# A two-layer kernel behind chunked attention: the first chunk's keys and values early, queries decayed by VectorE, states read by ScalarE

## The reference

```python
# q, k, v: 2 x 8 heads x 768 tokens x 64, float32
gamma = 1.0 - 2.0 ** (-5.0 - np.arange(H))
for t in range(S):
    state = gamma[None, :, None, None] * state + np.einsum('bhd,bhe->bhde', k[:, :, t], v[:, :, t])
    y[:, :, t] = scale * np.einsum('bhd,bhde->bhe', q[:, :, t], state)
# x = y as 1536 tokens x 512
h = x @ w_in                                # 512 -> 2048
x = (h * (1.0 / (1.0 + np.exp(-1.702 * h)))) @ w_out
rms = np.sqrt(np.mean(x * x, axis=-1, keepdims=True) + 1e-06)
xn = x / rms * rms_g
g = xn @ w_gate                             # 512 -> 1536
out = (g * (1.0 / (1.0 + np.exp(-g))) * (xn @ w_val)) @ w_out2
```

## Time and profile before

| | us |
|---|---|
| median of 3 runs | 584.25 |
| lowest and highest | 584.05, 584.41 |
| the profiled execution | 583.44 |
| its span, first to last instruction | 581.6 |
| TensorE busy in the span | 573.3 (99%) |
| VectorE, ScalarE, GpSimd busy | 359.2, 298.1, 172.1 |

### The profile page before, as it was taken

One profiled execution on the slowest core, in us unless ns is written; L12 is line 12 of the kernel. 1 busy time (PEld: TensorE's weight loads), 2 busy tenths in 40 slices (PEclk: granted clock), 3 DMA queues, 4 the chain that ended last, 5 costly groups with the idle time before them and its releaser, 6 DMA issues.

```text
span 581.6 us, 9400 instructions
## 1 busy us (share of the span) xinstructions
PE 573.3 (99%) x3640; PEld 551.8 (95%) x3640; DVE 359.2 (62%) x486; ACT 298.1 (51%) x501; POOL 172.1 (30%) x222
## 2 busy tenths in 40 slices
PE   7999999999999999999999999999999999999997
PEld 7988999999999999999999999998889999998886
DVE  5797555676425667775346768678755666666432
ACT  1244766645336766645237655574444555564321
POOL 2386444000222452000314464410051545420000
PEclk9999999999999999999999999999999999999999
DMA  8981222322112222312202222233213322224202
GB/s 319 392 292 37 74 72 73 108 73 73 38 36 73 72 74 70 111 39 72 73 0 74 73 74 72 74 84 99 73 36 125 93 73 73 73 74 112 69 1 108
DMA packets 24220, 52.84 MB, mean 91 GB/s; under 512 B 1776, under 2 KB 1904, under 8 KB 24176
## 3 DMA queue, kind: packets, MB, share of 16 engines
q1 hardware_dynamic: 23600, 50.41, 28.2%
q10 hardware_dynamic: 576, 1.84, 0.8%
HBM read 49.09 MB, written 3.15 MB: 90 GB/s over the span
## 4 chain that ended last, share of the span: by engine, by line
PE 97%; DVE 1%; DMA 1%; issue 0%; ACT 0%
PE bank L539 20%; PE twin L539 20%; PE twin L480 11%; PE twin L483 11%; PE twin L482 11%; PE bank L483 6%; PE bank L480 6%; PE bank L482 6%; PE twin L392 2%; PE bank L438 2%; PE bank L425 1%; DMA arena<-attn_in 1%; PE bank L409 1%; DVE x_lo L787 0%; PE bank L580 0%
## 5 line engine op out<-in xcount | busy, mean ns | idle before, releaser
L778 DVE TENSOR_TENSOR w_lo<-raw,w_hi 128x512 fp32r<-128x512 f32 (+2 forms) x148 | 149.3, 1024 | 49.7 <-ACT w_hi L612 49.5
L1059 POOL TENSOR_TENSOR raw<-raw 128x256 f32<-128x256 f32 x40 | 32.1, 803 | 317.1 <-DMA raw<-w 312.5
L480 PE MATMUL twin<-x_hi,w_hi 128*128 128x384 f32 x360 | 120.5, 335 | 0.6 <-ACT arena L676 0.6
L483 PE MATMUL twin<-x_hi,w_lo 128*128 128x384 f32 x360 | 120.3, 334 | 0.0
L482 PE MATMUL twin<-x_lo,w_hi 128*128 128x384 f32 x360 | 120.2, 334 | 0.0
L612 ACT ACTIVATE w_hi<-raw 128x512 fp32r<-128x512 f32 (+2 forms) x148 | 109.0, 763 | 18.0 <-PE bank L539 7.6
L813 DVE TENSOR_TENSOR g_lo<-arena,g_hi 128x768 fp32r<-128x768 f32 x56 | 54.3, 970 | 74.8 <-ACT g_hi L642 74.8
L642 ACT ACTIVATE g_hi<-arena 128x768 fp32r<-128x768 f32 x56 | 47.5, 848 | 103.6 <-PE bank L539 103.6
L480 PEld LDWEIGHTS twin<-x_hi,w_hi 128*128 128x128 f32 x360 | 67.6, 188 | 0.9 <-ACT arena L676 0.9
L482 PEld LDWEIGHTS twin<-x_lo,w_hi 128*128 128x128 f32 x360 | 67.6, 188 | 0.0
L483 PEld LDWEIGHTS twin<-x_hi,w_lo 128*128 128x128 f32 x360 | 67.6, 188 | 0.0
(11 more groups left out here) (105 smaller groups left out, 995.9 us busy)
## 6 DMA issues: line engine op xcount, KB each, us to landing
raw<-w SPq DMA_DIRECT2D x68, 512.0 KB, 3.7
arena<-attn_in SPq DMA_DIRECT2D x22, 512.0 KB, 7.9
out<-x SPq DMA_DIRECT2D x1, 1536.0 KB, 8.6
out<-x SPq DMA_DIRECT2D x6, 256.0 KB, 2.0
arena<-attn_in ACTq DMA_DIRECT2D x2, 512.0 KB, 10.1
arena<-tables ACTq DMA_DIRECT2D x1, 512.0 KB, 6.1
arena<-tables ACTq DMA_DIRECT2D x1, 256.0 KB, 9.8
ident<-ident_in SPq DMA_DIRECT2D x1, 64.0 KB, 12.8
```

What stands on the lines that cost most here:

```text
L480: pe.matmul(dst, w_hi[q][:, w], x_hi[:, x], start=start and kk == 0, stop=False, skip_group_check=True)
L483: mm = pe.matmul(dst, w_lo[q][:, w], x_hi[:, x], start=False, stop=kk == 1, skip_group_check=True)
L778: dve.tensor_tensor(w_lo[q % 3][:, dst], src, w_hi[q % 3][:, dst].bitcast(F32), ALU.subtract)\
L1059: pool.tensor_tensor(s1, a21, a22, ALU.add).then_inc(w_sums, 1)
```

## The change

The first chunk's queries come on SP's queue and its keys on ScalarE's, each 256 KB, and its keys and values in token order second on SP's; `load_kv(1)` and `load_kv(2)` change queues. Chunk 0 is finished (from_chunk, new_products) ahead of scores(1), with 12 fill matmuls before it in place of 3. `decay_q` is VectorE's for all chunks, right behind `masked`. `new_state` is ScalarE's: one instruction for chunks 0 and 6, and for the others four, one for each pair of heads. It stands ahead of `copy_y` and of most conversions in ScalarE's order. In the first hidden unit product 6 stands ahead of product 3, the split of T4 behind copy_u2, and the sum for T4 in the last attention round. Left out below are hunks that only rename a semaphore or write a wait's value by a helper.

```diff
--- before.py
+++ after.py
@@ -23,7 +23,7 @@
 NF1, NF2 = FF1 // P, FF2 // P
 EPS = 1e-6
 WARM_UP = 8
-FILL = 3
+FILL = 12
 T_MASK = HEADS + PAIRS
@@ -52,7 +52,7 @@
 UPPER = {True: (B11, B21, B22, T1, T3, T2, T4), False: (B11, B21, T1, T2, B22, T3, T4)}
-LOWER = {True: (B11, B21, T1, B22, T3, T2, T4), False: (B11, B21, T1, T2, B22, T3, T4)}
+LOWER = {True: (B11, B21, T1, B22, T2, T3, T4), False: (B11, B21, T1, T2, B22, T3, T4)}
 SET = ((0, 1, 2), (3, 4, 5))
...
@@ -318,6 +318,13 @@
                 ins = engine.memset(state_decay[64 * (h % 2):64 * (h % 2) + 64, at_:at_ + 1], gamma(h) ** (CHUNK * c))
             return ins
+        def qk_at(a):
+
+            return 16 * (a // SLOTS) + (32 if a % SLOTS == 0 else 16)
+
+        def kv_at(a):
+            return 16 * (a // SLOTS) + 16
+
         block = ctx.enter_context(nc.Block())
         @block.sync
@@ -339,9 +346,10 @@
                 sp.dma_start(dst, src).then_inc(raw_in[r % 2], 16)
-            load(0)
+            sp.dma_start(slot[0][:, 0:512], attn_in[0, :, 0:512]).then_inc(qk_in[0], 16)
+            load_kv(0)
             load(1)
-            load_kv(1)
+            load_kv(2)
             load(2)
             load(3)
             load_kv(3)
@@ -353,11 +361,13 @@
                     sp.wait_ge(scores_done, b - SLOTS + 1)
                     if (b - SLOTS) % CHUNKS > 0:
-                        g, c = chunk_of(b - SLOTS)
-                        sp.wait_ge(q_decayed[g], c)
+                        sp.wait_ge(q_decayed, cross_at(b - SLOTS) + 1)
                     load(b)
                 for b in (a, a + 1):
                     sp.wait_ge(y_done, b - SLOTS + 1)
+                    if b == SLOTS:
+
+                        sp.wait_ge(kv_done, 1)
                     load_kv(b)
                 if a == 8:
                     load_weights(1)
...
@@ -430,8 +439,7 @@
             def from_chunk(a):
                 par = a % 2
                 v = slot[a % SLOTS][:, 1536:2048]
-                if a % CHUNKS == CHUNKS - 1:
-                    pe.wait_ge(kv_in[a % SLOTS], 16 * (a // SLOTS) + 16)
+                pe.wait_ge(kv_in[a % SLOTS], kv_at(a))
                 pe.wait_ge(probs_done, a + 1)
                 for p in range(PAIRS):
                     for h in range(2):
@@ -442,19 +450,21 @@
                 mm.then_inc(y_done, 1)
             pe.wait_ge(ones_set, 1)
-            for _ in range(WARM_UP):
-                pe.matmul(gate[1][:, 0:P], ones[:, :], ones[:, :], start=True, stop=True)
+            def fill(count):
+
+                for _ in range(count):
+                    pe.matmul(gate[1][:, 0:P], ones[:, :], ones[:, :], start=True, stop=True)
+
+            fill(WARM_UP)
             for a in range(0, STEPS, 2):
                 scores(a)
                 if a == 0:
-
-                    for _ in range(FILL):
-                        pe.matmul(gate[1][:, 0:P], ones[:, :], ones[:, :], start=True, stop=True)
+                    fill(FILL)
+                    from_state(0)
+                    from_chunk(0)
+                    new_products(0)
                 scores(a + 1)
                 if a == 0:
-                    new_products(0)
-                    from_state(0)
-                    from_chunk(0)
                     from_state(1)
                     new_products(1)
                 else:
@@ -514,9 +524,9 @@
                     pe.wait_ge(m1_copied, n + 1)
                     product(2, n, 0, 0, 2, B21, False)
                     pe.wait_ge(w_lo_done, lo_at[r] + 2)
+                    product(6, n, 2, 1, 2, T2, False)
                     pe.wait_ge(m5_copied, n + 1)
                     product(3, n, 1, 1, 3, B22, False)
-                    product(6, n, 2, 1, 2, T2, False)
                 pe.wait_ge(u2_copied, n + 1)
                 pe.wait_ge(w_lo_done, lo_at[r] + 3)
                 product(7, n, 2, 1, 0, T3, False)
@@ -685,10 +695,10 @@
                    .then_inc(squared, 1)
+            act.dma_start(slot[0][:, 512:1024], attn_in[0, :, 512:1024]).then_inc(qk_in[0], 16)
             act.dma_start(mask, tables[:, T_MASK:T_Q]).then_inc(mask_in, 16)
-            act.dma_start(slot[0][:, 1024:2048], attn_in[0, :, 1024:2048]).then_inc(kv_in[0], 16)
             act.dma_start(q_table, tables[:, T_Q:T_ALL]).then_inc(q_table_in, 16)
-            act.dma_start(slot[2][:, 1024:2048], attn_in[2 * BATCH, :, 1024:2048]).then_inc(kv_in[2], 16)
+            act.dma_start(slot[1][:, 1024:2048], attn_in[BATCH, :, 1024:2048]).then_inc(kv_in[1], 16)
             act.wait_ge(ones_set, 1)
             act.activation(warm[:, :], ones[:, 0:1], ACT.Gelu_apprx_sigmoid)
@@ -700,6 +710,24 @@
                                gate[a % 2][:, :].rearrange("p (d k t) -> p d k t", d=2, k=2),
                                ACT.Copy).then_inc(y_copied, 1)
+            def new_state(a):
+                g, c = chunk_of(a)
+                if c == CHUNKS - 1:
+                    return
+                m = state_at(a)
+                act.wait_ge(kv_done, m + 1)
+                if m >= 2:
+                    act.wait_ge(cross_done, m - 1)
+                if c == 0:
+                    ins = act.activation(state[m % 2], val[g][:, 0:256], ACT.Copy)
+                else:
+                    for p in range(PAIRS):
+                        at_ = PAIRS * c + p
+                        ins = act.activation(state[m % 2][:, cols(p, 64)], val[g][:, cols(p, 64)], ACT.Copy,
+                                             scale=state_decay[:, at_:at_ + 1])
+                ins.then_inc(state_done, 1)
+
+            act.wait_ge(factors_set, 2)
             for a in range(0, STEPS, 2):
                 if a == 4:
                     split_x(0, B11)
@@ -709,13 +737,21 @@
                     split_x(0, B22)
                     split_w(0, 1)
                 elif a == 8:
-                    split_x(0, T1)
                     split_x(0, T3)
                     split_w(0, 2)
-                elif a == 10:
+                if a == 0:
+                    copy_y(0)
+                    new_state(0)
+                new_state(a + 1)
+                if a > 0:
+                    copy_y(a)
+                copy_y(a + 1)
+                if a + 2 < STEPS:
+                    new_state(a + 2)
+                if a == 6:
+                    split_x(0, T1)
+                elif a == 8:
                     split_x(0, T2)
-                copy_y(a)
-                copy_y(a + 1)
             for p, (layer, _) in enumerate(PHASES):
@@ -730,10 +766,10 @@
                     copy_m5(n)
                     if j > 0 and not is_val(n - 1):
                         activate(n - 1, 3)
+                    split_next(r, 0)
+                    copy_u2(n)
                     if n == 0:
                         split_x(0, T4)
-                    split_next(r, 0)
-                    copy_u2(n)
                     if not is_val(n):
                         activate(n, 0)
                     split_next(r, 1)
@@ -896,61 +932,39 @@
                 dve.tensor_tensor(prob[a % 2], twin[a % 2][:, :], mask, ALU.mult)\
                    .then_inc(probs_done, 1)
-            def new_state(a):
-                g, c = chunk_of(a)
-                if c == CHUNKS - 1:
-                    return
-                m = state_at(a)
-                dve.wait_ge(kv_done, m + 1)
-                if m >= 2:
-                    dve.wait_ge(cross_done, m - 1)
-                if c == 0:
-                    ins = dve.tensor_copy(state[m % 2], val[g][:, 0:256])
-                else:
-                    new, sums = (t.rearrange("p (k e) -> p k e", k=PAIRS) for t in (state[m % 2], val[g][:, 0:256]))
-                    ins = dve.tensor_tensor(new, sums, state_decay[:, cols(c, PAIRS)].unsqueeze(2).to_broadcast([P, PAIRS, 64]), ALU.mult)
-                ins.then_inc(state_done, 1)
-
             def decay_q(a):
-
                 r, x = a % SLOTS, cross_at(a)
                 if a == 1:
                     dve.wait_ge(q_table_in, 16)
-                dve.wait_ge(qk_in[r], 16 * (a // SLOTS) + 16)
+                dve.wait_ge(qk_in[r], qk_at(a))
                 if x >= 2:
                     dve.wait_ge(cross_done, x - 1)
-                dve.tensor_tensor(q_dec[x % 2], slot[r][:, 0:512], q_table, ALU.mult).then_inc(q_decayed[0], 1)
+                dve.tensor_tensor(q_dec[x % 2], slot[r][:, 0:512], q_table, ALU.mult).then_inc(q_decayed, 1)
             for a in range(0, STEPS, 2):
                 masked(a)
                 if a == 0:
                     decay_q(1)
-                    new_state(0)
                 masked(a + 1)
-                if a < 4:
-                    decay_q(a + 2)
-                elif a == 4:
+                for b in (a + 2, a + 3):
+                    if b < STEPS and b % CHUNKS > 0:
+                        decay_q(b)
+                if a == 4:
                     lower_x(0, B11)
-                elif a == 8:
-                    lower_x(0, T1)
```

(37 more changed lines are left out.)

## The result

| | before | after |
|---|---|---|
| median us (15 executions each) | 584.31 | 586.88 |
| lowest and highest | 583.52, 585.33 | 585.02, 590.36 |
| profiled execution, its span | 583.44, 581.6 | 585.10, 583.3 |
| TensorE, VectorE, ScalarE, GpSimd busy | 573.3, 359.2, 298.1, 172.1 | 574.3, 356.1, 306.0, 164.9 |

Ratio 1.0048, 95% interval [1.0037, 1.0059]: slower by 2.6 us, where 1.1 was forecast, and 0.1 us above the stated range. The profiled execution lies at the fast end and shows 1.7 of it. The 15 executions are not one cloud: those with a mean granted TensorE clock of 1.000 took 585.0 to 586.4, those with 0.997 took 586.5 to 588.4, those with 0.994 took 589.0 to 590.4. The medians of the three groups are 585.5, 587.2 and 589.6.

What follows compares the result with a forecast made beforehand. The prediction took TensorE's nearly gapless matmul stream as the bound, with key arrivals pinning the attention stage. Stage -0.2 and first unit +1.3 gave +1.1 us, 584.5 profiled, 0.8 more for the median: 585.3 us, range 583.0 to 586.8.

Steps and rivals of the forecast that it cites:

- The start: First chunk: scores from 5.2 us, clock rise at about 11.1, fills end at 11.7, chunk 2's scores at 17.1.
- The first chunk early: 0: Attention start: finishing the first chunk early changes the time by 0, ends -0.3 and +0.8 us.
- a gain is waited away: At chunk 4's keys: their arrival doesn't move, so TensorE's earlier time becomes waiting; a delay up to 0.34 us is absorbed.
- Rival 1: Attention stage: transfers come sooner, chunk 10's keys over 1.3 us before 42.54, stage -1.4 to -2.7, middle 583.5; chance 0.21.
- Rival 2: Attention start: too many fills, ending at 12.4, stage 0.8 us late, total +2.1, 586.3; chance 0.15.
- States and queries: Attention stage: states on ScalarE save the 0.28 us wait at 32.87 and 0.1 restart; queries on VectorE gain 0.1.
- The term that decides: First hidden unit: unit 1 waits for its weights and starts at 59.1 against 57.79, 1.3 us lost; ends 0.7 and 1.8.
- the T4 pair: First hidden unit, VectorE: lowering T4, then the next unit's first weights, taken as 2.48 us together.
- Rival 3: First hidden unit: the new wait isn't there, the unit saves 0.84 us, total 583.2; chance 0.09.
- The sum: Whole kernel: stage -0.2 and first unit +1.3 give +1.1 us, profiled execution 584.5, median 585.3.
- the median of the runs stands 0.8 above it: Last step: the median lies 0.8 us above the profiled execution, so 584.5 becomes 585.3.

Runs made afterwards that it cites:

- e1: The changed kernel with ScalarE's split of T4 put back before unit 1's first weight split and copy_u2: 583.98 us, ratio 1.0005.
- e4: The changed kernel with 3 fill matmuls instead of 12: 585.44 us.
- e8: The kernel before with product 6 ahead of product 3 in the first unit and nothing else: 583.42 us, ratio 0.9988.
- e6: The changed kernel with VectorE lowering unit 1's first weights ahead of T4: 583.75 us, ratio 0.9991.
- e3: The kernel before with product 6 ahead of product 3 and the split of T4 behind copy_u2: 585.57 us.
- e9: The changed kernel with one more 768-column VectorE subtraction ahead of the lowering of T4, lengthening the wait before unit 1: 589.18 us.
- e7: The changed kernel with the split of T4 put back and five idle matmuls each ahead of the products of chunks 4 and 10: 584.02 us.
- e10: The changed kernel with idle matmuls in all three long waits, nine ahead of unit 1, five each at chunks 4 and 10: 586.13 us.
- e11: The changed kernel with unit 1's weights lowered ahead of T4 and five idle matmuls each at chunks 4 and 10: 584.08 us, ratio 1.0002.
- e2: The changed kernel with nine idle matmuls before the wait for unit 1's w_lo: 585.67 us.
- e5: The changed kernel as it is, measured again as a yardstick on another chip: 585.89 us.

## Why the prediction was wrong

*The start.* The place of the scores was right (5.18 for 5.2), the clock wasn't. I let it rise at 11.1. The 24 fill records took 2.94 us, the same as in e1's profile, where the scores ahead of them already ran at the upper level (16 records in 1.16 us); so all of them ran at that level, the rise came by about 7.2, and the fills ended at 10.1 instead of 11.7. What stands between them and the scores of chunk 2 took 6.3 us (10.06 to 16.34) where I had 5.4, with waits of 0.20 and 0.24 us in it. The two errors partly cancel, which is luck. The step itself ("The first chunk early: 0") held because "a gain is waited away": the keys of chunk 4 absorbed it. Rival 1 fell, since chunk 10's keys came 0.34 us later and not sooner. Rival 2 fell with the fill end at 10.1, and e4 with three fills starts the scores of chunk 2 no sooner.

*States and queries.* Four state reads took 0.93 us for my 1.0, and the wait at 32.87 went. But one of the same size took its place. VectorE, with its conversions now ahead, comes 0.85 us later to the masks of chunks 6 and 7, and the from-chunk matmuls wait for it; before (first line) and after:

```profile
32.65 2.34 DVE L896 TENSOR_TENSOR arena<-twin,arena 128x1024 f32<-128x1024 f32 x2
```

```profile
33.50 2.34 DVE L932 TENSOR_TENSOR arena<-twin,arena 128x1024 f32<-128x1024 f32 x2
...
34.86 2.23 PE L446 MATMUL bank<-arena 128*64 128x128 f32 x32 [0.35 <-DVE arena L932]
```

By chunk 10's products TensorE was 0.74 us later than before (ready at 43.79 for 43.05), and the wait for the keys swallowed nearly all of it. The keys came at 42.88, 0.34 later than before, were decayed in 1.12 us for 1.38, and the stage ended 0.17 later, not 0.2 earlier.

In other profiles that decay is slower. In the new order it starts together with a pair of VectorE conversions; its rows, from e8 (order of before) and from e1 (order of the change):

```profile
43.09 1.04 POOL L1044 TENSOR_TENSOR arena<-arena 128x512 f32<-128x512 f32 x1 [2.77 <-DMA arena<-attn_in]
```

```profile
43.37 1.83 POOL L1057 TENSOR_TENSOR arena<-arena 128x512 f32<-128x512 f32 x1 [5.70 <-DMA arena<-attn_in]
```

Over the profiles it took 1.04, 1.04, 1.25 and 1.38 us in the old order and 1.05 to 1.83 in the new one. It also starts later: at 42.95 on average over four profiles of the old order, 43.39 over ten of the new. With the boundary clean on both sides and no idle matmuls, one pair compares the attention stages: 583.75 (e6) against 583.42 (e8), with intervals that overlap. So the changed stage is worth nothing; whether it costs a few tenths of a microsecond, and by which of the two, isn't shown.

*The first unit.* The term that decides was right in kind and in size: 1.3 forecast, 1.35 measured. Inside it two small errors cancelled, the T4 pair at 2.73 us for 2.48 and a restart of 0.06 us behind it for my 0.24. e1, e3 and e6 confirm the chain from three sides. Rival 3 fell.

*The sum.* For the profiled execution 584.5 was forecast and 585.10 came: 0.6 short, 0.4 of it from the stage and 0.14 from behind the boundary, where nothing was forecast. The failed step is the next one, "the median of the runs stands 0.8 above it": after the change it stood 1.8 above (586.88 against 585.10). The 0.8 was the distance of a kernel without a long pause in its matmuls; by carrying it over I priced the wait at its length alone and put the clock behind it at nothing, without a reason. What stood in its place is a second price, **some 1.6 us for each fall of TensorE's clock behind an idle wait**. By times and clocks it was paid in nine of fifteen executions, and about twice in three of them. I had looked at the clock only as something that rises once at the start; no rival let it fall. The Trainium skill ("TensorE: Matmul & The Clock Gate", What's actually happening) names falls after idleness, and I used none of it. In e4 a pause of 1.77 us went before one.

How far that is shown: e4 and e9 show the fall in its place and its cost in time; e7, e10 and e11 show none where the waits are filled or gone. That a longer wait brings more falls is only suggested by e9. e2, with only the boundary filled, still had one execution of eight at 588.1, and e1 three of twelve with only the key waits left, so the 1.2 to 1.7 us waits at chunks 4 and 10 probably take part; which of the waits caused which fall of the first measurement stays open, since only profiled executions show the place, and its own has no fall. In e5, with three executions of ten under clock 0.998, the same kernel took 585.89, 1.6 us above before and inside the range: there the forecast would have held by luck, with the same price missing.

## What to carry to other kernels

Before moving an instruction behind a copy, follow everything queued behind it on the next engine too: here a ScalarE edit delayed VectorE's first instruction in line and with it a second, unrelated one that TensorE waited for. Where TensorE never pauses, price a new pause of about 2 us twice, its length and the chance of a spell at half clock behind it. Where it can't be avoided, fill it with idle matmuls, but with fewer than the wait holds: at chunk 10 they overran the keys by about 1 us in e10's and e11's profiles. And a gain ahead of a wait for a transfer is no gain: the only part of this change that a run showed to be worth keeping was the swap of two products.

## What the runs showed of the hardware

- A pause of 1.77 us of TensorE was followed, 0.8 us after work had resumed, by 3.4 us at 1.2 GHz (e4's profile); one of 3.44 us by the same length, 0.4 us after work had resumed (e9's). Each cost 1.5 to 1.7 us of time.
- The same mean clock of 0.997 costs that or nothing, depending on where the fall lies (e4 against e8).
- With the same start of the kernel, the first scores ran at the lower level in one profiled execution (2.08 us at 6.73, before) and at the upper in another (1.16 us at 6.56, e8), so the start is not the same from one execution to the next.
